# Gated recurrent attention and an expert layer on one core: x made first in a chunk, tile rows gathered into three buffers

## The reference

```
m' = max(f + m, i);  fs = exp(f + m - m');  is = exp(i - m')
C = fs*C + is * v k^T;  n = fs*n + is*k
y = sigmoid(o) * (C q) / max(|n.q|, 1)            # x: 2 x 768 tokens of 320
logits = x @ w_gate;  local = sigmoid(x @ w_local)
e = argmax(logits) where local < 0.5 or s == 0, else the expert of the token before
out = softmax(logits)[e] * relu(x @ w1[e]) @ w2[e]  # w1 320x1024, w2 1024x320
```

## Time and profile before

| | us |
|---|---|
| median of 3 runs | 296.5 (295.55 to 296.61) |
| profiled execution | 297.23 |
| its span | 295.3 |
| PE busy | 263.5 (89%) |
| VectorE busy | 176.5 (60%) |
| ACT busy | 123.6 (42%) |
| POOL busy | 64.8 (22%) |

### The profile page before, as it was taken

One profiled execution on the slowest core, in us unless ns is written; L12 is line 12 of the kernel. 1 busy time (PEld: TensorE's weight loads), 2 busy tenths in 40 slices (PEclk: granted clock), 3 DMA queues, 4 the chain that ended last, 5 costly groups with the idle time before them and its releaser, 6 DMA issues.

```text
span 295.3 us, 5921 instructions
## 1 busy us (share of the span) xinstructions
PE 263.5 (89%) x2097; PEld 197.2 (67%) x2098; DVE 176.5 (60%) x358; ACT 123.6 (42%) x187; POOL 64.8 (22%) x86
## 2 busy tenths in 40 slices
PE   5899699989899899987699599999799999999990
PEld 1577588878788777763236588888676666666560
DVE  6588855397895957977791458888722332233220
ACT  2324634666766847634000346665523222333210
POOL 6073200504104010000021122333223233331111
PEclk9959955999999979996759799999999999999997
DMA  6997562658999881578717148841001010101000
GB/s 149 244 264 280 126 246 71 175 192 255 200 290 288 264 256 30 157 273 267 232 11 269 35 130 266 245 157 51 31 28 35 27 35 13 32 21 45 7 23 19
DMA packets 14305, 42.35 MB, mean 143 GB/s; under 512 B 3795, under 2 KB 5885, under 8 KB 14282
## 3 DMA queue, kind: packets, MB, share of 16 engines
q1 hardware_dynamic: 12314, 37.54, 42.8%
q0 software_dynamic: 1792, 4.34, 4.9%
q10 hardware_dynamic: 176, 0.17, 0.2%
HBM read 38.49 MB, written 4.99 MB: 147 GB/s over the span
## 4 chain that ended last, share of the span: by engine, by line
PE 46%; DVE 6%; DMA 2%; issue 1%; ACT 1%; POOL 0%; POOLq 0%; DVEq 0%
PE psU L927 17%; PE psS L907 9%; PE psO L893 5%; PE psS L893 4%; PE psO L914 2%; PE psS L701 2%; DMA xt<-x_rows,srcid 2%; PE psM L880 2%; DVE W L1220 1%; PE psU L872 1%; PE psM L744 1%; DVE W L1268 1%; PE psS L744 1%; PE psA L854 0%; ACT W L624 0%
## 5 line engine op out<-in xcount | busy, mean ns | idle before, releaser
L927 PE MATMUL psU<-W,hidT 128*128 128x320 f16 (+1 forms) x384 | 54.8, 299 | 0.4 <-DVE hidT L1352 0.4
L927 PEld LDWEIGHTS psU<-W,hidT 128*128 128x128 f16 x384 | 37.5, 98 | 14.7 <-issue 0.9
L788 PEld LDWEIGHTS psO<-W,hidT 128*128 128x128 f32 x192 | 28.1, 210 | 3.0 <-issue 1.1
L907 PE MATMUL psS<-W,xT 128*128 x128 | 28.9, 379 | 0.0
L502 POOL DMA_INDIRECT out<-rows,outid x16 | 16.2, 1010 | 56.7 <-DVE rows L1359 56.7
L766 PE MATMUL psS<-W 104*128 104x256 f32 x96 | 27.9, 428 | 0.0
L1336 DVE TENSOR_TENSOR xT<-psM,xT 128x384 f16<-128x384 f32 x16 | 8.9, 557 | 29.5 <-ACT xT L633 29.5
L633 ACT CAST xT<-psM 128x384 f16<-128x384 f32 x16 | 7.6, 476 | 44.5 <-PE psM L880 44.5
L1094 DVE TENSOR_TENSOR hidT<-psS,hid 128x512 f32<-128x512 f32 x24 | 16.5, 687 | 15.8 <-PE psS L766 15.5
L788 PE MATMUL psO<-W,hidT 128*128 128x41 f32 x192 | 25.9, 287 | 0.0
L468 POOL TENSOR_TENSOR W<-W 128x640 f32<-128x640 f32 x6 | 8.7, 1454 | 75.0 <-PE psU L832 65.0
(11 more groups left out here) (184 smaller groups left out, 480.1 us busy)
## 6 DMA issues: line engine op xcount, KB each, us to landing
W<-in_kvo SPq DMA_DIRECT2D x6, 968.0 KB, 7.2
stage<-in_w SPq DMA_DIRECT2D x9, 640.0 KB, 5.2
stage<-in_w SPq DMA_DIRECT2D x11, 512.0 KB, 4.6
W<-in_w SPq DMA_DIRECT2D x8, 512.0 KB, 5.8
W<-in_w SPq DMA_DIRECT2D x6, 640.0 KB, 5.6
rows<-in_w SPq DMA_DIRECT2D x5, 512.0 KB, 4.5
W<-in_qk SPq DMA_DIRECT2D x6, 416.0 KB
x_rows<-rows SPq DMA_DIRECT2D x12, 192.0 KB, 6.2
```

Source lines behind the costliest of these rows:

```text
L788: last = mm(own[j % 2][:, h], prob[j % 2][:, h], vb[u][:, QUAD * j + h], start=True, stop=True)
L907: last = mm(psS[:, half], x[:, k * P:(k + 1) * P], w, start=(n == 0), stop=(n == len(terms) - 1))
L927: last = mm(psU[:, 0:DM], h[:, k * P:(k + 1) * P], w, start=(k == 0 and n == 0), stop=(k == FC - 1 and n == 2))
```

## The change

In chunks 2 to 5 VectorE makes x and its scale's input ahead of both first weighings; weight splits stay between the other steps, logits are copied after the next x or before the third split. Chunk 1 has an order of its own on VectorE, ACT and PE, with the last gate factors transposed behind the fourth scores. Chunk 0's v is the first part of its load, with a semaphore of its own. The first eight tiles gather into three buffers (`xt` and two parts of `hid`); tile 0's x is transposed into psA and split into `hidT`, and tile 1's transposes stand in the middle of tile 0's product. Early late-lows are 5 (two of them behind the first tiles' splits), the others take 5 steps. A small gather of router weights runs on POOL before the first real one. The core of the diff:

```diff
-EARLY_LOWS = 3
-SPREAD_STEPS = 6
+EARLY_LOWS = 5
+SPREAD_STEPS = 5
...
+        xbufs = [xt[:], hid[:, 0:ROW], hid[:, ROW:2 * ROW]]
...
+        def x_buffer(t):
+            return t % 3 if isinstance(t, int) and t < E else 0
+        def tile_place(t):
+            if isinstance(t, int) and t == 0:
+                x = hidT[:].bitcast(F16)
+                return psA[:, 0], x[:, 0:KC * P], x[:, KC * P:2 * KC * P]
+            return psM[:], xh, xl
...  (SP)
+                if c == 0:
+                    sp.dma_start(kvob[u][:, 0:BH * V], kvo[c, :, 0:BH * V]).then_inc(s_v0, 16)
+                    sp.dma_start(kvob[u][:, BH * V:KVO_N], kvo[c, :, BH * V:KVO_N]).then_inc(s_kvo[u], 16)
+                    return
...
-                    sp.wait_ge(s_xl, 16)
+                    sp.wait_ge(s_xl[2], 16)
...  (POOL)
             pool.wait_ge(s_x, NC)
+            pool.indirect_dma_start(xt[:, 0:KC * (E + 1)], None, wr[:, :], ...).then_inc(s_warm, 16)
+            pool.wait_ge(s_warm, 16)
...
+                if isinstance(t, int) and t <= E + 1:
+                    users = [n for n in range(t) if x_buffer(n) == x_buffer(t)]
+                    wait_if(pool, s_xtr, users[-1] + 1 if users else 0)
+                    wait_if(pool, s_meta, users[-1] + 1 if users else 0)
...  (ACT, a chunk)
                 exponents(0)
...                  Cbd
+                exponents(1)
...                  chunk 1: e1, e2
                     split_high(A_CHUNK * (c - 1))
-                exponents(1)
-                act.wait_ge(s_kvo[c % 2], 16 * (c // 2 + 1))
-                wait_if(act, s_x, c)
-                nc.scalar.activation(th, ob[c % 2], ACT.Tanh, scale=0.5).then_inc(s_th, 1)
-                if c > 0:
+                if c > 1:
+                    keep_output_gate()
                     split_high(A_CHUNK * (c - 1) + 1)
                 exponents(2)
+                if c < 2:
+                    keep_output_gate()
...
                     x_evac(2 * (c - 1))
-                    keep_rows(c - 1, 0)
-                    split_high(A_CHUNK * (c - 1) + 2)
+                    if c == 1:
+                        split_high(1)
+                    else:
+                        split_high(A_CHUNK * (c - 1) + 2)
+                        keep_rows(c - 1, 0)
                 exponents(3)
+                if c == 1:
+                    split_high(2)
                 if c > 0:
                     split_high(A_CHUNK * (c - 1) + 3)
                     x_evac(2 * (c - 1) + 1)
+                    if c == 1:
+                        act.wait_ge(s_et, 3)
+                        keep_rows(0, 0)
                     keep_rows(c - 1, 1)
...  (PE, a chunk)
                 own_part(0)
                 exponents(2)
                 if c == 1:
-                    factors(2, NC)
-                if c > 0:
+                    own_part(1)
+                if c > 1:
                     x_transposes(2 * (c - 1), 0, c - 1)
                 scores(2)
+                if c == 1:
+                    x_transposes(0, 0, 0)
                 if c > 0:
                     old_part(1)
-                own_part(1)
+                if c != 1:
+                    own_part(1)
                 exponents(3)
...                  logits, scores(3)
+                if c == 1:
+                    pe.wait_ge(s_lg, 1)
+                    factors(2, NC)
                 own_part(2)
...  (PE, first tile)
                 for f in range(FC):
+                    if t == 0 and f == FC // 2:
+                        tile_transposes(1)
...  (VectorE, chunk 1)
+                    weigh(0); weigh(1); make_x(0); scale_old(0); combine(0); chunk_ends()
+                    weigh(2); combine(1); scale_old(1); split_low(0); keep_logits(0)
+                    weigh(3); chunk_decays(); make_scale(0); combine(2); split_low(1)
+                    decay_state(); split_low(2); add_state(); combine(3); split_low(3)
...  (VectorE, chunks 2 to 5)
+                make_x(c - 1)
+                keep_logits(2 * (c - 1) - 1)
                 weigh(0)
-                make_x(c - 1)
-                split_low(piece)
                 weigh(1)
                 scale_old(0)
                 combine(0)
+                split_low(piece)
                 make_scale(c - 1)
                 split_low(piece + 1)
                 weigh(2)
                 combine(1)
                 scale_old(1)
+                keep_logits(2 * (c - 1))
                 split_low(piece + 2)
-                keep_logits(2 * (c - 1))
                 weigh(3)
...
             make_x(NC - 1)
+            keep_logits(2 * (NC - 1) - 1)
             make_scale(NC - 1)
```

More of the change, by code:

```diff
@@ L506, in _ @@
                 gather(t)
+            for t in range(E - 1):
+                gather(t + 3)
+                write(t)
             n3 = tile_count(pool)
-            with pool.Fori(0, TILES - 3) as t:
+            with pool.Fori(E - 1, TILES - 3) as t:
                 with pool.If(t < n3):
@@ L631, in tile_high @@
                 act.wait_ge(s_xtr, t + 1)
-                wait_if(act, s_h, t)
-                nc.scalar.copy(xh, psM[:, 0:KC * P]).then_inc(s_xeh, 1)
+                if isinstance(t, int) and t == 0:
+                    act.wait_ge(s_rv, ROUTE_STEPS)
+                    act.wait_ge(s_pw, 16 * B)
+                elif not isinstance(t, int) or t > 1:
+                    act.wait_ge(s_h, t)
+                ps, h = tile_place(t)[0:2]
+                nc.scalar.copy(h, ps[:, 0:KC * P]).then_inc(s_xeh, 1)
             def first_hidden_high(t):
@@ L725, in x_transposes @@
                     pe.wait_ge(s_x, x_of + 1)
+                    pe.wait_ge(s_e12, 2)
+                else:
                     pe.wait_ge(s_dec, 1)
@@ L904, in up @@
                 for half in range(2):
-                    for n, (x, k, part) in enumerate(terms):
+                    for n, (x, k, part) in enumerate(terms(t)):
                         w = W1[:, bass.ds(e, 1), part, half * 512:(half + 1) * 512].rearrange("p a f -> p (a f)")
-                        last = mm(psS[:, half], x[:, k * P:(k + 1) * P], w, start=(n == 0), stop=(n == len(terms) - 1))
+                        last = mm(psS[:, half], x[:, k * P:(k + 1) * P], w, start=(n == 0),
+                                  stop=(n == len(terms(t)) - 1))
                 last.then_inc(s_h, 1)
@@ L1133, in step, with decay_state, add_state @@
                 piece = A_CHUNK * (c - 1)
+                def decay_state():
+                    dve.wait_ge(s_c, c)
+                    vv.tensor_tensor(Ctmp, Cst, dec[:, c, :, None].to_broadcast([P, BH // 2, V]),
+                                     ALU.mult).then_inc(s_ct, 1)
+                def add_state():
+                    dve.wait_ge(s_ct, c)
+                    dve.wait_ge(s_u, c + 1)
+                    dve.wait_ge(s_cbd, 2 * c + 2)
+                    vv.tensor_tensor(Cst, Ctmp, Uv, ALU.add).then_inc(s_c, 1)
+                if c == 1:
+                    weigh(0)
+                    weigh(1)
+                    make_x(0)
+                    scale_old(0)
+                    combine(0)
+                    chunk_ends()
+                    weigh(2)
+                    combine(1)
+                    scale_old(1)
+                    split_low(0)
+                    keep_logits(0)
+                    weigh(3)
+                    chunk_decays()
+                    make_scale(0)
+                    combine(2)
+                    split_low(1)
+                    decay_state()
+                    split_low(2)
+                    add_state()
+                    combine(3)
+                    split_low(3)
+                    return
+                make_x(c - 1)
+                keep_logits(2 * (c - 1) - 1)
                 weigh(0)
-                make_x(c - 1)
-                split_low(piece)
                 weigh(1)
@@ L1362, in _ @@
             tile_low(1)
+            for n in range(EARLY_LOWS - 2, EARLY_LOWS):
+                late_low(n)
             def first_step(t, late):
```

95 lines of the change are left out of this document (56 added, 39 removed).

## The result

The changed kernel takes 270.22 us (median of 4 runs, 268.85 to 271.70) against 296.02 (295.01 to 296.61) for the kernel before, timed beside it: ratio 0.913 (0.906 to 0.920), 25.8 us less. The profiled execution of the changed kernel took 268.93. Single runs of one kernel spread with the clock that they were granted (the kernel before, in other runs, from 287.6 us at clock 0.941 to 303.1 at 0.894; the changed kernel's slowest of 14 took 275.4), so what follows compares medians of all runs of a kernel, and traces stretch by stretch.

The account below looks back on a forecast made before the run. PE was taken to pace attention, with chunk 1 ten us out of line at low clock. Terms 12.0 + 6.6 + 0.3 + 5.0 + 1.6 = 25.5, less 1.7 and 0.8: 23.0; 297.2 to 274.2, less 0.7: 273.5 us, range 267 to 285.

Parts of the forecast that it names:

- Chunks 0 and 1: First two attention chunks: 3.0 us from an earlier start, 9.0 from chunk 1's own order; 12.0 won together.
- 0.8 us lost at L1005: VectorE in chunk 0: loss beside POOL's `kS` product stays; moving VectorE's work earlier only picks another victim.
- (a): Chunk 1: weight piece 3 loads only after `split_low(0)`, ACT's split and x copy wait; PE loses about 0.9 us.
- (b): Start of chunk 2: ACT's rows and query stacking delay exponentials and `Cbd`; PE's old part waits about 1.3 us.
- Chunks 2 to 5: Attention: waits for `scale_old` 3.7, for logits' copies 1.2, chunk 4's low clock 1.7; 6.6 us won, bounds 0 to 8.
- The transfers: Chunks 2 to 4: 0.8 us deducted for late DMA; rival that transfers bound them, +3 to +4, 277, chance 0.14.
- The 1.7 for one fall: Deduction of 1.7 us for one fall of the clock at (a) or (b).
- sign of being wrong: Chunks 1 to 5: a stretch at clock 0.50 longer than 7 us would show the prediction wrong.
- the 5 to 8 of the rival: Rival that the clock stays low in chunk 1: +5 to +8 us, 280, chance 0.17.
- The tiles: Expert part's first tiles: three row buffers put tile 1's product 3.9 us after tile 0's; 5.0 us won before `down(0)`.
- Late lows: Last expert: five early lows in five steps remove its 1.5 us wait; 1.6 with gaps, bounds 0 to 1.7.
- End of attention and routing: `make_x(5)` starts 0.5 us earlier, less 0.2 for a copy: 0.3 won; routing unchanged, 0 to 0.9 by the clock.

Follow-up runs that it names:

- before_fill: The kernel before with 12 idle filler matmuls on PE ahead of chunk 1's wait for the factors: 285.35 us against 296.40.
- no_c1: The changed kernel with chunk 1's order of before on VectorE, ACT and PE: 281.99 us, +11.6.
- all_three: The changed kernel with ACT's query stacking earlier, chunk 2's weighing ahead of x, 14 fillers instead of 20 and an earlier last logits copy: 268.61 us.
- stack_early: The changed kernel with ACT stacking chunk 2's queries ahead of the weight piece it waits for: 270.25 us against 269.93.
- after_again: The changed kernel run once more, unaltered, as the measure for other runs: 270.35 us; the kernel before in those turns 295.89.
- no_c25: The changed kernel with VectorE's order of before in chunks 2 to 5, ACT's order staying new: 280.42 us, +10.1.
- no_v: The changed kernel with chunk 0's keys, values and gates in one transfer again: 270.19 us, no difference between the medians.
- lows36: The changed kernel with three early lows and six steps, as before: 275.68 us, about +5.3.
- no_tile: The changed kernel with the gathers, tile places and early lows of before: 276.16 us against 270.35.
- only_tile: The kernel before with only the change's gathers, tile places and early lows: 290.90 us against 296.40.

## Why the prediction came out, step by step

The forecast was 273.5 and the median 270.2, just inside the forecast's own range (270 to 277.5); of the changed kernel's other medians, 270.35 and 269.93, one lies outside it. The mechanisms came as described, but the sizes were too small in sum, and that the total is near is owed in part to errors that cancel. Against its own terms, in the profiled executions:

*Chunks 0 and 1.* 12.0 forecast; own part 0 of chunk 2 moved from 58.89 to 45.98, 12.9, of which 0.8 lies ahead of chunk 0 and is none of the change's. The round took 19.3 against 18.9. As forecast: the weighing came early, the 2.2 and 0.73 went, the clock stayed up, and before_fill and no_c1 show that it was the stall that had brought it down: 6.6 of 10.4 us are the clock. v apart, costed with chunk 0, has no gain of its own that the medians show.
Two sizes in it were wrong and in part cancel. PE's work in the round was put at chunk 2's 16.5; but chunk 1 has the factor products besides, and takes 17.45 us without a wait, where chunks 3 to 5 take 16.12. And own part 0 of chunk 1 came at 26.69 instead of 28.0, with the 0.8 of the earlier start in it, and chunk 0's VectorE lost nothing beside POOL: the prediction said that 0.8 us lost at L1005 would stay, but POOL's `kS` product began at 24.35, behind the gates, and the gates' instruction at that place (L1080, 22.05) took 0.69 and not 1.57. So the collision did not pick another victim in that chunk. One of VectorE's three idle pieces there (the 0.52 at 15.13) had also stood ahead of the low clock, and not in it.

*(a) and (b).* Both mechanisms are there, and their sizes are off. (a) 0.9 was forecast, 0 came in this execution, because piece 3 landed in 3.8 us and was issued 1.3 earlier than I put it; all_three's trace has 1.57. (b) 1.3 was forecast, 0.76 came, and 0.87 behind it, which I did not name: by chunk 2's start VectorE has fallen behind, with a split of 1.79 us and all of `make_x` (2.7 us) ahead of the weighing. stack_early shows that (b) hardly counts, and that VectorE does. The sum of both, 2.2 forecast and 1.6 measured, was near for a partly wrong reason.
The split's 1.79 us stand against a mean of 1.48 for its kind in the kernel before; POOL's `kS` product ran beside its first 0.44 us (39.69 to 41.16, the split from 40.72). The Trainium skill ("SBUF — State Buffer", "Who interferes with whom"), whose rule the prediction weighed, would make that a loss of at most 0.44: the trace agrees, with 0.31. In after_again the product ran beside the first 0.73 us, and the split took 2.08, 0.60 more than the mean.

*Chunks 2 to 5.* 6.6 forecast, 8.1 measured from own part 0 of chunk 2 to the end of chunk 5. Here a term was mis-sized: I priced each wait at its listed idle time. Scores 2 and the old part behind them in chunk 3, before and after:

```profile
78.41 1.03 PE L766 MATMUL psS<-W 104*128 104x256 f32 x4
80.43 1.09 PE L777 MATMUL psU<-W 104*128 104x82 f32 x8 [0.99 <-DVE W L1102]
```

```profile
64.12 1.03 PE L825 MATMUL psS<-W 104*128 104x256 f32 x4
64.98 1.02 PE L836 MATMUL psU<-W 104*128 104x82 f32 x8
```

They start 2.02 apart before and 0.86 after. So a listed wait of 0.99 cost 1.16 us between these two starts, and another 0.07 by the next: as the trace lists them, matmuls that don't wait overlap in their ends (the profile models these ends), and that overlap is lost too. In the same way 0.23 listed for the copy of logits cost 0.43. A chunk without waits is 16.12, not the 16.5 that I took; four chunks of it make the missing 1.5. no_c25 says the same from the other side: 2.1 and 1.8 us for 1.67 and 1.41 listed.

*The transfers.* 94% busy took nothing in chunks 2 to 4: PE waits for none of them, ACT and POOL do. The 0.8 I took off for it was wrong, and the rival falls. The step that failed is to read the busy share as a fixed load of 16.7 us a chunk: chunk 3 moved 4.7 MB in 16.7 us of busy share before (264 GB/s over 17.77 us) and 4.5 MB in 14.7 after (277 over 16.13).

*The clock.* The 1.7 for one fall didn't come in this execution. It does come in others with chunk 1's own order: 3.4 us low in after_again, no_v (chunk 1) and all_three, 10.2 in lows36 (from chunk 1 into chunk 2), so taking something off was right. The last is longer than the 7 us which the prediction gave as a sign of being wrong; it cost chunk 1 some 3.0 us (20.47 against 17.45, both cut at the chunk's first matmul), and not the 5 to 8 of the rival. That this rival stayed out of the medians is in part the luck of the runs. Its own sum is also 8.5 - 1.3 - 0.9 - 1.7 = 4.6, a little under the +5 that it names.

*The tiles.* 5.0 forecast, 4.9; 3.9 between the products, 3.91; no_tile and only_tile give 5.8 and 5.5 with the lows. Warming the gather can have bought nothing on PE, as forecast: row 0 lay ready at 133.6 and the fillers ran to 135.3.

*Late lows.* 1.6 forecast, 1.7 between the traces; undone, the runs ask 4.0 for it, since the wait brings the low clock with it.

*End of attention and routing.* 0.3 forecast, 0.9. The 0.3 are there. The other 0.6 are where the low clock lay: it covered the last logits' product before (L744, 1.54 us at 132.21) and not after (L803, 0.93 at 110.90), though the mean clock of the stretch is nearly the same (0.73 and 0.72).

Without deductions that is 25.5 forecast and 28.5 measured in the traces; with them 23.0, against 25.8 between the medians.

## What to carry to other kernels

Price a stall of TensorE at its listed idle time, plus the overlap of the matmuls around it, plus the half speed that may follow; in chunk 1 here the last was the largest of the three. When a long stage shows a low clock, put idle matmuls over its longest wait first: one cheap run and its trace tell how much is the clock and how much the order (here 6.6 and 3.8 us in chunk 1). Where two waits of one engine follow each other, look at what holds the later one before you shorten the earlier: the earlier may be only its cover, as ACT's was over VectorE's, and shortening it alone gave nothing.

## What the runs showed of the hardware

The granted clock can fall and stay low while PE has no wait that the trace lists. In lows36 chunk 1 shows 20.66 us with 20.66 busy, and the clock was low for 10.24 us from 36.3 on, with PE busy for all of them, in a kernel whose same instructions ran at 1.00 in other executions. Once down it stayed down 17.0 us in the kernel before and 23.9 in no_c1, with PE 96% busy in the former.

A gather by POOL that begins inside a VectorE instruction with two inputs in SBUF waits for it. In the rows of the first tiles above, VectorE's pair of lows at 129.92 takes 1.18 each; the gather that began ahead of them took 1.01, the one that began in the second, at 131.16, took 1.99 and ended 0.87 behind it. The same in no_tile, which has no warming gather:

```profile
130.75 2.36 DVE L1284 SCALAR_TENSOR_TENSOR W<-stage,W 128x1024 f16<-128x1024 f32 x2
130.99 2.09 POOL L499 DMA_INDIRECT xt<-x_rows,srcid  x1 [21.04 <-DVE eid L1388]
```

It began in the first of the pair, which ended at 131.93, and itself ended 1.15 behind that. The 0.28 more are likely those of a first gather. In no_c25 the warmed gather of tile 0 too began inside VectorE's first low, which ended at 142.30, and ended 0.93 behind it; the warming one, with VectorE in no instruction when it began, took 1.23:

```profile
126.22 1.23 POOL L501 DMA_INDIRECT xt<-in_wr,gid  x1 [27.16 <-issue]
...
141.61 1.62 POOL L526 DMA_INDIRECT xt<-x_rows,srcid  x1 [8.70 <-DVE eid L1434]
```

1.23, against 1.00 for the others; it gathers another tensor, so that the 0.2 are those of the first use is likely and not shown. So of the 2.09 us of the first gather in the kernel before, about 1 was the wait for VectorE and 0.2 to 0.3, by this estimate, the first use, and warming takes only the latter. The Trainium skill (the section cited above) has a VectorE instruction with two SBUF inputs contend with a GpSimd instruction that reads SBUF, and a gather reads its row numbers there: these traces agree. The same is seen on a plain POOL instruction: the bf16 copy at 41.23 of the changed kernel's trace, begun inside the split of 40.72 to 42.51, took 1.54 us, where its kind takes 0.39 to 0.42 in most other places. No run kept the late lows away from the gathers, so what that would give is left open; the fillers cover it here.
